# Two-stage mixture of experts on one core: the second routing's logits as eight extra columns of the down products, and Pool's subtractions in pieces

## The reference

```python
# first mixture
logits = x @ w_gate                  # capacity 384 rows per expert
h = np.maximum(x[mask] @ w1[e], 0.0); out[mask] = h @ w2[e]      # 320 -> 1024 -> 320
# second mixture, x is now that output
xn = x / (np.linalg.norm(x, axis=-1, keepdims=True) + 1e-06)
en = expert_emb / (np.linalg.norm(expert_emb, axis=-1, keepdims=True) + 1e-06)
logits = xn @ en.T / tau
expert_idx = np.argmax(logits, axis=1)
gate_w = softmax(logits)[expert_idx]
out[mask] = gate_w[mask, None] * (np.maximum(x[mask] @ w1[e], 0.0) @ w2[e])
```

## Time and profile before

| | us |
|---|---|
| timed runs | 1056.11, 1055.52, 1050.94; median 1055.52 |
| profiled execution, its own time | 1052.89 |
| its span | 1051.0 |
| PE busy | 768.7 (73%) |
| DVE busy | 572.6 (54%) |
| POOL busy | 392.9 (37%) |
| ACT busy | 216.4 (21%) |
| mean granted TensorE clock | 0.827 |

### The profile page before, as it was taken

How to read it: one execution, slowest core, us unless ns; L and a number is a source line. 1 busy time by engine, 2 the same in 40 slices (tenths; PEclk the granted TensorE clock), 3 DMA queues, 4 the chain that set the end, 5 groups by cost and what they waited for, 6 DMA issues and landing times.

```text
span 1051.0 us, 18901 instructions
## 1 busy us (share of the span) xinstructions
PE 768.7 (73%) x5803; PEld 683.1 (65%) x5804; DVE 572.6 (54%) x1591; ACT 216.4 (21%) x451; POOL 392.9 (37%) x334
## 2 busy tenths in 40 slices
PE   1989998893233333205989999998399999898996
PEld 1777786782122222205989989987288898787995
DVE  7786678647867667711376666576523222222221
ACT  3222222100000000001323423323033333222331
POOL 4443333134300000071365654466314444443741
PEclk9997789996555555556988998898599999998998
DMA  5453345165400000032576667674645556556220
GB/s 139 126 153 117 112 127 148 24 193 176 150 0 0 0 0 0 0 119 77 182 226 196 210 198 232 196 229 144 193 118 177 178 159 205 192 155 183 90 98 1
DMA packets 70227, 137.26 MB, mean 131 GB/s; under 512 B 14791, under 2 KB 53968, under 8 KB 66098
## 3 DMA queue, kind: packets, MB, share of 16 engines
q1 hardware_dynamic: 43282, 67.16, 21.4%
q0 software_dynamic: 11008, 58.16, 16.7%
q10 hardware_dynamic: 15904, 11.53, 4.3%
HBM read 77.36 MB, written 14.48 MB: 87 GB/s over the span
## 4 chain that ended last, share of the span: by engine, by line
PE 38%; DVE 18%; issue 10%; DMA 8%; POOL 6%; ACT 1%; SPq 0%; DVEq 0%; ACTq 0%; POOLq 0%
DMA w_hi<-w_raw 8%; PE bank L1307 5%; PE bank L1308 4%; PE bank L1309 4%; PE bank L1293 4%; PE bank L1330 2%; PE bank L1262 2%; POOL w_lo L634 2%; PE bank L1331 2%; PE bank L1332 2%; POOL w_lo L652 2%; PE bank L1364 2%; DVE routing_arena L859 2%; DVE routing_arena L892 2%; DVE routing_arena L954 2%
## 5 line engine op out<-in xcount | busy, mean ns | idle before, releaser
L1307 PE MATMUL bank<-w_hi,hT_hi 128*128 (+1 forms) x440 | 146.2, 332 | 8.2 <-issue 2.6
L1308 PE MATMUL bank<-w_lo,hT_hi 128*128 (+1 forms) x440 | 141.0, 320 | 0.0
L1309 PE MATMUL bank<-w_hi,hT_lo 128*128 (+1 forms) x440 | 140.8, 320 | 0.0
L606 POOL DMA_INDIRECT x_sorted<-tokens,routing_arena x48 | 47.4, 988 | 192.0 <-DVE routing_arena L942 164.2
L1293 PE MATMUL bank<-routing_arena 128*8 128x16 bf16 x1344 | 43.2, 172 | 103.2 <-DVE routing_arena L859 103.2
L652 POOL TENSOR_TENSOR w_lo<-w_raw,w_hi 128x2560 fp32r<-128x2560 f32 x16 | 91.1, 5692 | 72.9 <-DMA w_hi<-w_raw 72.4
L1293 PEld LDWEIGHTS bank<-routing_arena 128*8 128x8 bf16 x1344 | 37.5, 94 | 108.3 <-DVE routing_arena L859 108.3
L634 POOL TENSOR_TENSOR w_lo<-w_raw,w_hi 128x2048 fp32r<-128x2048 f32 x16 | 73.0, 4564 | 72.3 <-DMA w_hi<-w_raw 71.5
L1307 PEld LDWEIGHTS bank<-w_hi,hT_hi 128*128 128x128 f32 x440 | 87.5, 199 | 11.6 <-issue 11.4
L1308 PEld LDWEIGHTS bank<-w_lo,hT_hi 128*128 128x128 f32 x440 | 87.5, 199 | 0.0
L1309 PEld LDWEIGHTS bank<-w_hi,hT_lo 128*128 128x128 f32 x440 | 87.2, 198 | 0.0
(11 more groups left out here) (253 smaller groups left out, 1808.8 us busy)
## 6 DMA issues: line engine op xcount, KB each, us to landing
w_raw<-in_moe_w SPq DMA_DIRECT2D x16, 1280.0 KB, 6.7
w_hi<-w_raw POOLq DMA_DIRECT2D x16, 1280.0 KB, 8.4
w_raw<-in_moe_w SPq DMA_DIRECT2D x16, 1024.0 KB, 7.8
w_hi<-w_raw POOLq DMA_DIRECT2D x16, 1024.0 KB, 4.6
w_hi<-w_raw POOLq DMA_DIRECT2D x32, 256.0 KB, 6.1
mlstm_arena<-in_q SPq DMA_DIRECT2D x64, 120.0 KB
routing_arena<-x_sorted ACTq DMA_DIRECT2D x31, 160.0 KB, 2.2
w_raw<-in_moe_w SPq DMA_DIRECT2D x16, 256.0 KB, 8.6
```

Of the source, the lines that this page charges most:

```text
L606: pool.indirect_dma_start(dst, bass.IndirectOffsetOnAxis(ap=dest[:, g:g + 1], axis=0), tokens[:, slot, :], None).then_inc(scattered, 16)
L1307: T.matmul(dst, a_hi, b_hi, start=first, stop=False)
L1308: T.matmul(dst, a_hi, b_lo, start=False, stop=False)
L1309: return T.matmul(dst, a_lo, b_hi, start=False, stop=last)
```

## The change

Four things move together.

1. w2_hi and w2_lo get 8 more columns (YW = 328): w2[e] times the normalised embeddings. PE makes them in the first routing (`emb_products`, 24 fp32 products of 8 columns per expert: two behind each round's L1298, the last 8 behind the phase's ranks, expert 7's behind the last ranks). For it the host hands in a transposed copy of w2, which SP loads in 16 halves ahead of expert 2's weights; ACT copies the result, POOL's `gate_columns` splits it in hi and lo behind each w2_lo. down3's products are 328 wide, and the raw logits come out of the same bank as the result (`raw3`). turn_results3, logits3 and xl_copies3 are gone, as is the copy L954 (ACT makes it now).
2. On DVE, choose3(e-1) stands directly behind x_lo3(e+1), ahead of the results; place3 ahead of result3(e, 2). On PE ranks3(e-1) stands between down3(e, 1) and down3(e, 2), in bank 2. ACT makes the squares of expert e at the end of its own step and root and exponential of e-1 behind the row loads.
3. POOL's subtractions come in pieces, for all 16 experts: w1_lo in 4, the third in 2, w2_lo in 4. w2_hi is moved into 8 strips of 320 of its 328 columns.
4. The embeddings are normalised within the loop of the first logits and no longer under the scatter. Results of the first experts go to the tokens' own blocks, not to a ring of six.

```diff
-                nc.gpsimd.tensor_tensor(w1_lo[:, s, :, :], w1_raw[:, 0:2, :], w1_hi[:, s, 0:2, :], ALU.subtract).then_inc(w1_ready, 1)
+                for k in range(2):
+                    for h in range(2):
+                        c = slice(h * HF, (h + 1) * HF)
+                        last = nc.gpsimd.tensor_tensor(w1_lo[:, s, k, c], w1_raw[:, k, c], w1_hi[:, s, k, c], ALU.subtract)
+                last.then_inc(w1_ready, 1)
                 pool.wait_ge(w1_ready, 2 * n + 1)
-                nc.gpsimd.tensor_tensor(w1_hi[64:128, s, 2, :], w1_raw[64:128, 2, :], w1_hi[64:128, s, 2, :], ALU.subtract).then_inc(w1_ready, 1)
+                for h in range(2):
+                    c = slice(h * HF, (h + 1) * HF)
+                    last = nc.gpsimd.tensor_tensor(w1_hi[64:128, s, 2, c], w1_raw[64:128, 2, c], w1_hi[64:128, s, 2, c], ALU.subtract)
+                last.then_inc(w1_ready, 1)
...
-                pool.dma_start(w2_hi[:, s, :, :], w2_raw[:, :, :]).then_inc(hi2_ready, 16)
+                pool.dma_start(w2_hi[:, s, :, 0:DM], w2_raw[:, :, :]).then_inc(hi2_ready, 16)
...
-                nc.gpsimd.tensor_tensor(w2_lo[:, s, :, :], w2_raw[:, :, :], w2_hi[:, s, :, :], ALU.subtract).then_inc(w2_ready, 1)
+                for k in range(0, FT, 2):
+                    c = slice(k, k + 2)
+                    last = nc.gpsimd.tensor_tensor(w2_lo[:, s, c, 0:DM], w2_raw[:, c, :], w2_hi[:, s, c, 0:DM], ALU.subtract)
+                last.then_inc(w2_ready, 1)
+
+            def gate_columns(n):
+                s = n % RING
+                nc.gpsimd.tensor_copy(w2_hi[:, s, :, DM:YW], w2e[:, n, :, :]).then_inc(w2g_hi, 1)
+                pool.wait_ge(w2g_hi, n + 1)
+                nc.gpsimd.tensor_tensor(w2_lo[:, s, :, DM:YW], w2e[:, n, :, :], w2_hi[:, s, :, DM:YW], ALU.subtract).then_inc(w2g_ready, 1)
...
+            def emb_products(e, first, last_m):
+
+                for m in range(first, last_m):
+                    f, k = m // KT, m % KT
+                    h, at = f // (FT // 2), k * HF + f % (FT // 2) * 128
...
+                    last = T.matmul(bank[3][:, ds(e * FT * E + f * E, E)], w2t[h][0:KP[k], at:at + 128], eg[0:KP[k], k * E:(k + 1) * E],
+                                    start=(k == 0), stop=(k == KT - 1))
...
                     T.matmul(bank[7][:, 8:8 + E], kcol[:, 0:1].to_broadcast([E, 128]), kscale[:, r, :], start=True, stop=True).then_inc(kb_ready, 1)
+                    emb_products(ph, 2 * r, 2 * r + 2)
...
-                dst, cols = bank[5 + b][:, 0:DM], slice(b * 128, (b + 1) * 128)
+                dst, cols = bank[5 + b][:, 0:YW], slice(b * 128, (b + 1) * 128)
...
                 down3(e, s, 0)
-                if route:
-                    turn_results3(e - 1, 1 - s, e + 2 if more else E)
                 down3(e, s, 1)
                 if route:
-                    logits3(e - 1, BPE * e + 1)
+                    ranks3(e - 1, e + 2 if more else E)
                 down3(e, s, 2)
-                if route:
-                    ranks3(e - 1)
...
                 if not isinstance(e, int) or e < E - 1:
-                    x_lo3(e + 1, 1 - p)
+                    x_lo3(e + 1)
                 route = not isinstance(e, int) or e > 0
                 if route:
-
-                    dve.wait_ge(scattered, 16 * (G + BPE * (e - 1)))
-                result3(e, p, 0)
+                    choose3(e - 1)
+                result3(e, 0)
+                result3(e, 1)
                 if route:
-                    xl_copies3(e - 1)
-                result3(e, p, 1)
-                if route:
-                    choose3(e - 1)
-                result3(e, p, 2)
-                if route:
-                    place3(e - 1, 1 - p)
+                    place3(e - 1)
+                result3(e, 2)
```

More of the change, by code:

```diff
@@ L167, in build @@
         w1_lo = sb("w1_lo", [128, RING, KT - 1, F], fp32r)
[L168 to L169 removed]
+        w2_hi = sb("w2_hi", [128, RING, FT, YW], fp32r)
+        w2_lo = sb("w2_lo", [128, RING, FT, YW], fp32r)
         w1_raw = sb("w1_raw", [128, KT, F])
@@ L436, in x_hi3 @@
             def x_hi3(e):
+                act.wait_ge(xt3_ready, KT * e + 1)
+                nc.scalar.activation(tokens[:, ds(BPE * e, BPE), DM], rows[:, :, XROW - 2], ACT.Copy).then_inc(ids3_ready, 1)
                 for k in range(KT):
@@ L665, in _ @@
                 scatter(x_sorted, g, g)
+            pool.wait_ge(w2e_ready, 1)
+            for n in range(RING):
+                gate_columns(n)
             for n in range(RING, E + RING):
@@ L1050, in experts1 @@
+                result3(e, 2)
+            def experts1():
+                x_lo3(0)
+                step3(0)
+                base, per = chain.n, 18 + BPE
+                with dve.Fori(1, E - 1) as e:
+                    chain.ahead = (e - 1) * per
+                    step3(e)
                     assert chain.n - base == per, chain.n - base
-                chain.n, chain.ahead = base + per * (E // 2 - 1), 0
-                step3(E - 1, 1)
-                xl_copies3(E - 1)
+                chain.n, chain.ahead = base + per * (E - 2), 0
+                step3(E - 1)
@@ L1271, in logits @@
                         product(g - 1)
+                    if g == G - 6:
+                        pe.wait_ge(emb_ready, 1)
+                        for k in range(KT):
+                            last = T.transpose(bank[3][0:KP[k], k * E:(k + 1) * E], emb[:, k * 128:k * 128 + KP[k]], ident[0:E, 0:E])
+                        last.then_inc(embT_ready, 1)
                 product(G - 1)
@@ L1465, in experts2 @@
                 down(NB2 - 1)
-            pe.wait_ge(emb_ready, 1)
-            for k in range(KT):
-                last = T.transpose(bank[3][0:KP[k], k * E:(k + 1) * E], emb[:, k * 128:k * 128 + KP[k]], ident[0:E, 0:E])
-            last.then_inc(embT_ready, 1)
-            pe.wait_ge(embT_done, 1)
             experts1()
@@ L1529 @@
         arrays[name] = np.ascontiguousarray(inputs[name])
+    w2t = np.zeros((E, 2, 128, KT, HF), np.float32)
+    for k in range(KT):
+        part = inputs["moe_w2"][:, :, k * 128:k * 128 + KP[k]].reshape(E, 2, HF, KP[k])
+        w2t[:, :, 0:KP[k], k, :] = part.transpose(0, 1, 3, 2)
+    arrays["moe_w2t"] = w2t.reshape(E, 2, 128, W2T)
     arrays["moe2_tau"] = np.asarray(inputs["moe2_tau"]).reshape(1)
```

189 lines of the change are left out of this document (100 added, 89 removed).

## The result

The changed kernel took 1071.34 us (median of four, 1069.5 to 1076.78), before beside it 1053.23; the ratio is 1.018 [1.013, 1.024]. The forecast was 1070, 1036 to 1086, slower. The number fits. Most of its terms do not, and on another chip six runs of the same kernel took 1046 to 1077, with a median 1.005 of before's. The ratios with an interval leave out runs more than 1.5% above the fastest of their kernel, which are three of six in c1 and four of six in e5, so there the median of all is given too.

The account below looks back on a forecast made before the run. PE was taken to bound the first experts, with small waits for a DVE that POOL makes late. Terms 16.3 - 3.3 + 0.2 + 0.5 - 0.7 + 3.5 = +16.5 on 1052.9 gave 1069.4, forecast 1070 us, range 1036 to 1086.

Parts of the forecast that it names:

- One DVE operation per seam: Between POOL's subtraction pieces one waiting DVE operation gets the ports, two where POOL waits on itself.
- Where the burst lies: First experts: POOL's gapless subtractions start 2.3 us behind an expert's up products, so choose3 ends at 16.0 us.
- the five intervals: First experts, ends of up products from expert 2 to 7: 33.9 us each against 30.6, together +16.3 us.
- X(0) to X(1): From the end of expert 0's up products to expert 1's: 72 products with 8 columns more, +0.2 us.
- X(1) to X(2): End of expert 1's up products to expert 2's: choose3 finishes in POOL's DMA wait, 31.3 against 34.6, -3.3 us.
- X(7) to the last row number: Behind expert 7's up products: the same wait, less the turns and logits, +0.5 us.
- the table's part: DVE's table chain between first and second experts meets one w2_lo as before, now in pieces: 0.
- Rival (a): POOL lets several DVE operations through at each seam, PE never waits, intervals 24.0 us: 1010 us in all, chance 0.15.
- First routing: Shorter port waits in phase 0 against embedding products in each round: sum -0.7 us.
- phases behind phase 0: First routing: embedding products add 0.05 us a round over 56 rounds, +2.8 us, bounds 0 and 17.
- phase 0: Start of the first routing: POOL's pieces shorten DVE's waits, -3.5 us (-1 to -6).
- Second experts: Serial weight chain: piece starts 0.05 us each, 0.3 an expert, w2_hi's strip move 0.4: +3.5 us (1 to 12).

Follow-up runs that it names:

- c1: The changed kernel once more, on another chip: median of six runs 1059.01 us, 1.005 of before's; its first three runs alone 0.993.
- e5: The changed kernel with w2_hi and w2_lo of the second mixture packed without the 8 columns: median of six runs 1059.38 us, 1.005 of before's.
- c0: The kernel before once more, unchanged, on the same chip as c1: one run, 1063.25 us.
- e1: The kernel before with w2_hi's rows padded to 328 columns, so its move goes in 8 strips a partition: 1089.38 us, ratio 1.011.
- e2: The kernel before with POOL's subtractions in pieces for all 16 experts, nothing else: 1077.99 us, ratio 0.998.

## Why the prediction was right, and where it was not

The number was right through terms that cancel. I go through them.

- **One DVE operation per seam**: right but for the copy L1062, which shared a seam with a neighbour at each of the five steps (e = 1 to 4 and 6) where the burst met it.
- **Where the burst lies**: this step failed. "At X+2.3 POOL starts a burst without a gap" was read from before and carried over to a kernel whose intervals and moves differ. In the changed kernel the burst started at X+6.6, 3.5, 2.3, 2.3, 2.3 and 5.6, and had a gap of 0.9 to 1.9 us between w2_lo and w1_lo where it started early, in which six operations passed at X(2). With it choose3 ended at X+10.9 to 15.2 instead of 16.0, and the five intervals took 151.1 us, -2.0 against before and not +16.3. At e = 3, 4 and 5 the start was the forecast's own X+2.3, and the intervals were 32.2, 30.6 and 28.0 against 33.9: there it is the gap that the forecast lacked. The longest, 33.1, had the burst at X+3.5.
- **The smaller terms**: X(0) to X(1) was +1.4 for +0.2, 0.84 of it a wait of PE for a hidden lo part. X(1) to X(2) was -4.2 for -3.3; by the forecast's own terms, with choose3 at X+12.8 and not 16.0, it should have read 30.7 and -3.9. X(7) to the last row number was -6.0 where I had +0.5, and the table's part +1.9 where I had 0.
- **Rival (a)**, intervals of 24.0: they came, at 23.9, in c1, though not by POOL letting operations through. choose3 runs before the burst starts. The time had a chance of 0.15, and the forecast listed the condition ("if DVE reaches choose3 with POOL already done") without its mirror, POOL not yet begun. In the two traces the modes part over 0.2 us in the landing of a load at e = 1, which a seam and the clock made 3.5 us.
- **First routing**: phases behind phase 0 took 26.58 and not 26.07, +3.1 for the six, forecast +2.8 for all seven; phase 0 -2.1, forecast -3.5 within -1 to -6, though c1's phase 0 is only 0.1 below c0's. With the logits ahead of it the stage came to +0.4 for -0.7. Right in kind and near in size.
- **Second experts**: mis-sized, +13.5 for +3.5, beyond the stated bound of 12 (which by its own parts, 2.5 and 0.3 on five experts, is 14). Seams cost 0.14 us each and not 0.05, 1.0 an expert; the strips 1.9 (issue 0.37, landing 1.5), where the forecast took 0.4 and had 2.5 as the upper bound; what is left of the 3.5 us a turn is in w1's landing and is not told apart. e1 and e2 show each alone. The Trainium skill's "DMA: Bandwidth & Descriptors" (Why small descriptors are slow) says a move inside SBUF doesn't pay for small descriptors; e1 measured +11 us from strips of 1280 bytes in place of rows of 10240, so here the measurement decides, against the page. The Trainium skill's "SBUF — State Buffer" (Who interferes with whom) stood: two-input products and one-input copies and scalings waited, the reciprocal L857 and the reduction L1058 took 0.18 us under a piece, and with the burst held back the waits at X(1) to X(4) were gone.
- **Attention**: +11.4 in this trace, in no term. It goes with the clock, and c0 has +9.5 of it without the change; in how far the change adds to it is open.

The forecast's 1070 came out by luck: errors of -18 us in the five intervals and -6.5 behind X(7) met +10 in the second experts and +11 in the attention. That all four runs of the first measurement were in the long mode is seen in one trace only; the other three times, 1069.8 to 1076.8, fit it. Had the short group of c1 been the measurement, 1046 to 1050, the kernel would have come out at 0.993 of before and not at 1.018.
